# The first block's filter divided at rounding, its taps split over three engines, and other orders for tiles 0 to 30

## The chip, the cores and the metric

One core of one Trainium2 chip runs the whole program. The metric is the device time of one execution in microseconds (us); lower is better. The program is written out instruction by instruction for each engine: TensorE (PE; its weight loads are PEld), VectorE (DVE), ScalarE (ACT), GpSimd (POOL) and SyncE (SP, which issues most DMAs). Each engine runs its own list in order, and semaphores tie the lists together.

## What is computed

A short causal filter over the sequence, whose seven taps per head are a softmax, then two feed-forward layers with gates of their own:

```python
w = np.exp(weight - max); w = w / (np.sum(w, axis=-1, keepdims=True) + 1e-09)   # 8 heads x 7 taps
x = filter of x with w, causal, over S = 4096 for B = 2 sequences, D = 192      # 8192 tokens x 192
h = x @ w_in                                   # layer 1: 192 -> 2048
g = h * np.clip(h + 3.0, 0.0, 6.0) / 6.0
x = g @ w_out                                  # 2048 -> 192
h = x @ w_in2                                  # layer 2: 192 -> 2048
P = a[0] + a[1]*h + a[2]*h**2 + a[3]*h**3
Q = 1.0 + abs(b[0])*abs(h) + abs(b[1])*h**2
out = (P / (Q + 1e-6)) @ w_out2                # 2048 -> 192
```

## The kernel before, in words

The 8192 tokens are 16 blocks of 512, and features stand on the partitions. The 192 features are split into 128 (part a) and 64 (part b). A layer has 16 tiles of 128 hidden features per block, so each layer has 256 tiles. Every float32 operand of a product is kept as a rounded high part and a remainder (`_hi`, `_lo`): one ACT copy rounds, and a subtraction on POOL or DVE gives the remainder. A tile is five matmuls of 512 columns into the hidden features (`in_product`: a high times high, a low weight times high, a high weight times low, and two for part b, whose high and low halves are stacked) and five out of them (`out_product`). 2 layers x 256 tiles x 10 = 5120 matmuls. Between the two stand the gate of layer 1 (ACT `relu1`, DVE `gate1`, ACT `g1hi`, then `g1lo` on DVE before tile 21 and on POOL after it) or the quotient of layer 2 (nine ACT, DVE and POOL operations). Four PSUM banks `h_0` to `h_3` hold hidden tiles.

Layer 2 of a block runs 20 tiles behind layer 1. Tile counters `p` (layer 1) and `s` (layer 2) advance in `course`, and for each step `run` walks a list of stages from a table: START, BEGIN, RAMP (from tile 20 on, when layer 2 joins), MIDDLE, and others at the end. An entry as `("out1", 4)` places a stage that many tiles late; the order of the entries is the order of the instructions on that engine. So the tables alone set what stands behind what.

The filter: for block 0, part a is seven taps on DVE, added one after the other into a PSUM bank that is not yet in use (`conv_a_tap`, which is `sums_a(0)`). Part b is seven half-width products on ACT (`product_b`), added on POOL (`add_lower_taps`) and DVE (`add_upper_taps`, `add_halves`). The taps are a softmax: DVE finds the maximum (L893), ACT takes the exponentials with their sum (L870), and DVE adds 1e-9, inverts and scales (`normalize`) before the first tap. Beside the taps DVE refines a square root of |b1| in small steps (`refine`), which layer 2 needs in a register. `cs_a_hi`, `cs_a_lo`, `cs_b_hi`, `cs_b_lo` split the filtered block into the parts that TensorE reads. `w_in_hi`, `w_in_lo`, `w_out_hi`, `w_out_lo` do so for the weights, chunk by chunk (two tiles each). TensorE runs eight spare products (L860) while it waits for the first block. Then tiles 0 to 3 run their three part-a matmuls first, and after them their part-b ones.

Of the kernel before, what the change touches and what calls it, by code (L numbers as in the profile page):

```python
# [11 lines left out]
P = 128  # L12
BLK = 512
# [3 lines left out]
Q_ONE = 1.0 + 1e-6  # L17

TAPS_READY = 6

SPLIT_B = 4
# [39 lines left out]
    "tensor": [("in2", 0), ("in1", 0), ("out2", 4), ("out1", 2)],  # L61
    "scalar": [("conv_a_first", AHEAD, -2), ("w_out_hi", -2), ("rsq2", 1), ("w_in_hi", -2), ("relu1", 0),
             ("rec2", 1), ("sq2", 0), ("abs2", 0), ("lin2", 0), ("g2hi", 2), ("g1hi", 0), ("cs_a_hi", AHEAD, 9)],
    "vector": [("num2", 1), ("conv_a", AHEAD, (2, 4, 3, 5, 7, 8)), ("g1lo", 2), ("num1", 1), ("g_neg", 2),
             ("gate1", 0), ("newton", 1), ("conv_b_tail", AHEAD, (9, 11, 13), 0), ("g_first", 1)],
    "gpsimd": [("x2a_lo", SUM1, -1), ("den_sum", 0), ("w_in_lo", -4), ("w_out_lo", 7), ("g1lo", 0),
# [38 lines left out]
START_END, RAMP_END, END_AT = 11, 30, 258  # L105
WARM = 8
# [10 lines left out]
def build_program(nc, x_a, x_b, taps, coefs, w_pack, out):  # L117
# [56 lines left out]
    with ExitStack() as ctx:  # L174
# [811 lines left out]
```

## Time and profile before

| what | value |
| --- | --- |
| median of 3 runs | 1207.81 us (1207.76 to 1207.96) |
| the profiled execution | 1206.88 us, of which its span 1205.1 us |
| granted TensorE clock over the span | 0.999 |
| TensorE matmul busy | 1177.9 us (98%), 5138 matmuls |
| DVE, ACT, POOL busy | 1161.2, 1169.7, 1075.7 us (96%, 97%, 89%) |
| chain that ended last | TensorE 91%, ACT 5% |

A matmul row shows about 0.39 us from start to modelled end, but back-to-back matmuls start 0.227 us apart, since they are pipelined; a wait shows as a larger distance between starts. The tables below give such starts. A busy share is an average; the stretches of the first group of rows show where TensorE had gaps.

### The profile page before, as it was taken

What the parts mean: (1) busy time and instruction counts of PE and PEld (TensorE: products, weight loads), DVE (VectorE), ACT (ScalarE), POOL (GpSimd) and SP (SyncE); (2) the same over time, 40 slices, a digit from 0 to 9 for tenths busy, and PEclk for the clock granted to TensorE, in tenths of its full rate; (3) what the DMA queues carried; (4) which work ended last, traced back from release to release, by engine and by line L of the source; (5) the groups of instructions that cost most, each with busy time, mean ns of one, the idle gap of its engine ahead of it and who ended that gap; (6) DMA issues with size and microseconds to landing.
All of it is one profiled execution on the core that took longest, in us unless ns stands there. A gap on an engine that the chain in (4) does not pass through costs nothing.

```text
span 1205.1 us, 18313 instructions
## 1 busy us (share of the span) xinstructions
PE 1177.9 (98%) x5138; PEld 963.0 (80%) x5138; DVE 1161.2 (96%) x1787; ACT 1169.7 (97%) x2233; POOL 1075.7 (89%) x832
## 2 busy tenths in 40 slices
PE   6999999999999999999999999999999999999987
PEld 5778888888888888888888888888888888888764
DVE  7899999999999999999999999999999999999898
ACT  7899999999999999999999999999999999999998
POOL 5879989999999999999899998999989999898876
PEclk9999999999999999999999999999999999999999
DMA  4400000000000000010000000000000000000000
GB/s 149 149 1 10 1 23 1 23 10 23 1 1 28 5 23 1 1 32 1 23 1 22 11 1 23 1 23 10 1 23 1 23 1 13 2 1 14 1 14 14
DMA packets 10021, 21.17 MB, mean 18 GB/s; under 512 B 1600, under 2 KB 1856, under 8 KB 9920
## 3 DMA queue, kind: packets, MB, share of 16 engines
q1 hardware_dynamic: 9632, 20.00, 5.6%
q8 instruction: 40, 0.66, 0.2%
q14 instruction: 61, 0.50, 0.1%
q10 hardware_dynamic: 288, 0.01, 0.0%
HBM read 13.72 MB, written 6.29 MB: 17 GB/s over the span
## 4 chain that ended last, share of the span: by engine, by line
PE 91%; ACT 5%; issue 2%; DVE 1%; DMA 0%; POOL 0%; ACTq 0%; DVEq 0%; POOLq 0%
PE h L321 46%; PE y0a_acc L333 5%; PE y0b_acc L339 5%; PE y0a_acc L335 5%; PE y0a_acc L334 5%; PE y0b_acc L338 5%; PE y1a_acc L333 4%; PE y1b_acc L339 4%; PE y1b_acc L338 4%; PE y1a_acc L335 4%; PE y1a_acc L334 4%; ACT g_hi L532 1%; ACT num L440 1%; ACT den L446 0%; ACT sqr L452 0%
## 5 line engine op out<-in xcount | busy, mean ns | idle before, releaser
L469 POOL TENSOR_TENSOR den<-den,sqr 128x512 f32<-128x512 f32 x246 | 360.6, 1466 | 92.8 <-ACT den L446 88.5
L526 POOL TENSOR_TENSOR g_lo<-g,g_hi 128x512 fp32r<-128x512 f32 x255 | 334.0, 1310 | 2.8 <-ACT g_hi L532 2.8
L433 POOL TENSOR_TENSOR g_lo<-r,g_hi 128x512 fp32r<-128x512 f32 x235 | 306.0, 1302 | 4.2 <-ACT g_hi L532 2.4
L463 DVE SCALAR_TENSOR_TENSOR num<-num,coef,h 128x512 f32<-128x512 f32 x246 | 183.8, 747 | 8.3
L496 DVE SCALAR_TENSOR_TENSOR h<-num,coef,h 128x512 f32<-128x512 f32 x238 | 178.1, 748 | 0.2
L458 DVE TENSOR_TENSOR num<-num,h 128x512 f32<-128x512 f32 x246 | 167.8, 682 | 9.6 <-ACT num L440 4.4
L440 ACT ACTIVATE num<-h,coef 128x512 f32<-128x512 f32 x246 | 176.2, 716 | 0.2
L473 ACT ACTIVATE rsq<-den 128x512 f32<-128x512 f32 x246 | 158.6, 645 | 11.5 <-POOL den L469 8.5
L532 ACT ACTIVATE g_hi<-g 128x512 fp32r<-128x512 f32 x255 | 168.0, 659 | 1.8 <-DVE g L503 0.4
L419 DVE SCALAR_TENSOR_TENSOR r<-r,h 128x512 f32<-128x512 f32 x235 | 160.7, 684 | 6.1 <-ACT r L412 5.0
L489 DVE SCALAR_TENSOR_TENSOR den<-den,h 128x512 f32<-128x512 f32 x238 | 161.7, 680 | 0.6 <-ACT h L485 0.3
L503 DVE SCALAR_TENSOR_TENSOR g<-den,h 128x512 f32<-128x512 f32 x238 | 161.7, 679 | 0.2
L532 ACT ACTIVATE g_hi<-r 128x512 fp32r<-128x512 f32 x235 | 156.4, 665 | 0.0
L412 ACT ACTIVATE r<-h 128x512 f32<-128x512 f32 x256 | 154.4, 603 | 1.4 <-PE h L321 1.4
L446 ACT ACTIVATE den<-h 128x512 f32<-128x512 f32 x246 | 151.4, 615 | 2.0 <-DVE g L503 2.0
L452 ACT ACTIVATE sqr<-h 128x512 f32<-128x512 f32 x246 | 149.9, 609 | 0.6
L485 ACT ACTIVATE h<-rsq 128x512 f32<-128x512 f32 x240 | 147.4, 614 | 0.9 <-DVE conv_b L463 0.2
L333 PE MATMUL y1a_acc<-g_hi,wout 128*128 128x512 f32 x254 | 100.2, 395 | 8.7 <-POOL g_lo L526 6.2
L321 PE MATMUL h<-x1a_hi,win_hi 128*128 128x512 f32 x256 | 100.4, 392 | 2.7 <-DVE g L503 2.3
L333 PE MATMUL y0a_acc<-g_hi,wout 128*128 128x512 f32 x256 | 100.1, 391 | 2.4 <-DVE g_lo L433 1.4
L321 PE MATMUL h<-x0a_hi,win_hi 128*128 128x512 f32 x256 | 100.7, 393 | 0.9 <-ACT x0a_hi L532 0.4
L321 PE MATMUL h<-x1a_lo,win_hi 128*128 128x512 f32 x256 | 100.0, 391 | 0.7 <-POOL x1a_lo L540 0.7
(151 smaller groups left out, 2982.4 us busy)
## 6 DMA issues: line engine op xcount, KB each, us to landing
stage_w<-w_pack SPq DMA_DIRECT2D x16, 448.0 KB, 3.4
raw_a<-x_a SPq DMA_DIRECT2D x16, 259.0 KB, 3.3
out<-y_a SPq DMA_DIRECT2D x16, 256.0 KB, 2.0
out<-y_b SPq DMA_DIRECT2D x16, 128.0 KB, 2.3
raw_b<-x_b SPq DMA_DIRECT2D x14, 129.5 KB, 2.7
raw_b<-x_b SPq DMA_DIRECT2D x4, 65.5 KB, 4.1
tap_ab<-taps ACTq DMA_DIRECT2D x1, 7.0 KB, 3.0
coef<-coefs ACTq DMA_DIRECT2D x1, 3.0 KB, 4.0
```

The lines of the kernel that those rows point to most:

```text
L321: mm = eng.matmul(psum, w, x[:, :], start=(i == 0), stop=(i == len(passes) - 1))
L333: eng.matmul(ya_acc[l][:, :], a_hi, g_hi[:, :], start=first, stop=False)
L433: eng.tensor_tensor(g1_lo[t % 2][:, :], gated(t)[:, :], f32(g1_hi[t % 2][:, :]), ALU.subtract).then_inc(S["g1lo"], 1)
L440: eng.activation(num_of(t), h2_of(t), ACT.Identity, bias=a2, scale=reg_a3) \
L458: eng.tensor_tensor(n, n, h2_of(t), ALU.mult).then_inc(S["num2"], 1)
L463: eng.scalar_tensor_tensor(out=n, in0=n, scalar=a1, in1=h2_of(t), op0=ALU.add, op1=ALU.mult).then_inc(S["num1"], 1)
L469: eng.tensor_tensor(den_of(t), den_of(t), sqr_of(t), ALU.add).then_inc(S["den_sum"], 1)
L489: eng.scalar_tensor_tensor(out=den_of(t), in0=den_of(t), scalar=Q_ONE, in1=quotient(t), op0=ALU.add, op1=ALU.mult).then_inc(S["newton"], 1)
L496: eng.scalar_tensor_tensor(out=raw_quotient(t), in0=num_of(t), scalar=a0, in1=quotient(t), op0=ALU.add, op1=ALU.mult).then_inc(S["g_first" ...
L503: eng.scalar_tensor_tensor(out=g2[t % 2][:, :], in0=den_of(t), scalar=2.0, in1=raw_quotient(t), op0=ALU.subtract, op1=ALU.mult) \
L526: eng.tensor_tensor(g2_lo[t % 2][:, :], g2[t % 2][:, :], f32(g2_hi[t % 2][:, :]), ALU.subtract).then_inc(S["g2lo"], 1)
L532: return eng.activation(dst, src, ACT.Copy)
```

## The change

**The first block's filter is divided later.** DVE's taps and ACT's products of block 0 use the exponentials as they are (`exp_tap`). The reciprocal of their sum is multiplied in when the filtered block is rounded (`cs_a_hi`, `cs_b_hi` as a scaled copy) and when its remainder is taken. The scaled taps go to a buffer of their own, `tap`, after that, for the other blocks.

**Two of part a's seven taps move to ACT.** `product_a` makes the products of taps 5 and 6, POOL adds them to each other (`add_products_a`), and DVE adds the pair to its five taps (`last_of_a`). Part b's seven products are shared out as three for POOL and four for DVE, where they were four and three.

**The square root leaves DVE.** It is taken by ACT in seven small steps, with the function `Abs_reciprocal_sqrt` and one correction, from tile 4 on; the three register loads come after it at tile 8.

**Spare products.** 24 instead of 8, on a tile of ones that POOL makes at the very start, so they wait no longer for weights.

**Orders.** Tiles 0 and 1 run their two high part-a passes, then their low ones; tiles 2 and 3 their low pass just before part b. SP issues the first weight chunk after part b of the input. START, BEGIN and RAMP list their stages in other orders; from tile 30 on nothing is reordered.

```diff
-TAPS_READY = 6
-SPLIT_B = 4
+SPLIT_A, SPLIT_B = 5, 3
+SUMS_READY, TAPS_READY = 5, 7
...
 RAMP = {
-    "tensor": [("in2", 0), ("in1", 0), ("out2", 4), ("out1", 2)],
+    "tensor": [("in1", 0), ("in2", 0), ("out1", 2), ("out2", 4)],
...
-START_END, RAMP_END, END_AT = 11, 30, 258
-WARM = 8
+START_END, RAMP_END, END_AT = 12, 30, 258
+WARM = 24
...
                 if t == 0:
-                    for tile in range(H_BANKS):
+                    for parts in (range(2), range(2, 3)):
+                        for tile in range(WCHUNK):
+                            first_block_weights(eng, 0, tile, "w_in_done")
+                            in_product(eng, 0, tile, h1_of(tile), split, parts)
+                    for tile in range(WCHUNK, H_BANKS):
                         first_block_weights(eng, 0, tile, "w_in_done")
-                        in_product(eng, 0, tile, h1_of(tile), split, range(3))
-                in_product(eng, 0, t, h1_of(t), split, range(3, 5)).then_inc(S["h1_done"], 1)
+                        in_product(eng, 0, tile, h1_of(tile), split, range(2))
+                rest = range(3 if t < WCHUNK else 2, 5)
+                in_product(eng, 0, t, h1_of(t), split, rest).then_inc(S["h1_done"], 1)
...
+        def product_a(eng, j):
+            if j == SPLIT_A:
+                eng.wait_ge(d_raw[0], 16)
+                eng.wait_ge(S["setup_s"], 1)
+            scaled(eng, sqr[j - SPLIT_A][:, :], raw_a[0][:, j:j + BLK], exp_tap[0][:, j:j + 1]) \
+                .then_inc(S["product_a"], 1)
+        def add_products_a(eng):
+            eng.wait_ge(S["product_a"], 2)
+            eng.tensor_tensor(sqr[0][:, :], sqr[0][:, :], sqr[1][:, :], ALU.add).then_inc(S["product_a"], 1)
+        def last_of_a(eng):
+            eng.wait_ge(S["product_a"], 3)
+            eng.wait_ge(S["conv_a_tap"], SPLIT_A)
+            eng.tensor_tensor(sums_a(0), sqr[0][:, :], sums_a(0), ALU.add).then_inc(S["conv_a_tap"], K - SPLIT_A)
...
+            if k == 0:
+                eng.wait_ge(S["setup_v"], SUMS_READY)
+                ins = scaled(eng, xa_hi[0][0][:, :], sums_a(0), tap_sum[:, 0:1])
...
+        def root_begin(eng):
+            eng.wait_ge(d_const, 16)
+            eng.activation(beta[:, :], coef[:, 4:6], ACT.Abs).then_inc(S["root"], 1)
+            eng.wait_ge(S["root"], 1)
+            eng.activation(r, b1_abs, ACT.Abs_reciprocal_sqrt, bias=B_TINY).then_inc(S["root"], 1)
...
         def registers(eng):
-            eng.wait_ge(S["root_done"], 1)
+            eng.wait_ge(S["root"], 7)
...
         @block.sync
         def _(eng):
             load_a(eng, 0)
-            load_w(eng, 0)
             for right in range(2):
                 load_b_half(eng, 0, right)
-            for c in range(1, W_STAGES):
+            for c in range(W_STAGES):
                 load_w(eng, c)
...
         @block.tensor
         def _(eng):
-            eng.wait_ge(S["wi_hi"], 1)
+            eng.wait_ge(S["ones"], 2)
+            ones = xa_hi[1][0]
             for _ in range(WARM):
-                eng.matmul(h1_of(H_BANKS - 1), win_hi[0][:, 0:P], win_hi[0][:, 0:BLK], start=True, stop=True)
+                eng.matmul(h1_of(H_BANKS - 1), ones[:, 0:P], ones[:, :], start=True, stop=True)
...
         @block.vector
         def _(eng):
...
+            eng.wait_ge(S["setup_s"], 1)
+            sums = invert(0) + invert(1)
+            for j in range(SPLIT_A):
                 conv_a_tap(eng, 0, j)
+                if j < len(sums):
+                    eng.wait_ge(*((S["setup_v"], n_own[0]) if j % 2 else (S["setup_s"], 1 + j // 2)))
+                    own(sums[j]())
...
+            last_of_a(eng)
+            for j in range(SPLIT_B + 1, K):
                 add_upper_taps(eng, j)
             add_halves(eng)
+            cs_a_lo(eng, 0)
             cs_b_lo(eng, 0)
+            for part in range(2):
+                normalize(part)
...
         @block.gpsimd
         def _(eng):
-            w_in_lo(eng, 0)
+            eng.memset(rsq[0][:, :], 1.0).then_inc(S["ones"], 1)
+            eng.wait_ge(S["ones"], 1)
+            eng.tensor_tensor(xa_hi[1][0][:, :], rsq[0][:, :], rsq[0][:, :], ALU.mult).then_inc(S["ones"], 1)
+            add_products_a(eng)
             for j in range(1, SPLIT_B):
                 add_lower_taps(eng, j)
+            w_in_lo(eng, 0)
             w_in_lo(eng, 1)
```

Where instructions stand now, at the three places of which the prediction speaks. On POOL, the start of the program before (`win_lo` are weight remainders, `num` part b's products):

```order
L540 ISA
L540 TENSOR_TENSOR win_lo<-stage_w,win_hi 128x512
L657 TENSOR_TENSOR num<-num 128x256 x3
L540 TENSOR_TENSOR win_lo<-stage_w,win_hi 128x512 x2
L540 TENSOR_TENSOR wout<-stage_w,wout 128x2x128
```

and now (`rsq` and `x1a_hi` are the buffers that hold the ones, `sqr` the two products of part a):

```order
L999 MEMSET rsq 128x512
L1001 ISA
L1001 TENSOR_TENSOR x1a_hi<-rsq 128x512
L671 TENSOR_TENSOR sqr<-sqr 128x512
L688 TENSOR_TENSOR num<-num 128x256 x2
L550 TENSOR_TENSOR win_lo<-stage_w,win_hi 128x512 x3
```

The first weight remainder moved behind the ones and three additions, and one of part b's additions left POOL. On ACT, behind the exponentials, before (`num`, `den`, `y0b_acc` take part b's products; `y1b_acc` the root):

```order
L873 ACTIVATE beta<-coef 128x2
L875 ACT_TABLE_LOAD
L875 ACTIVATE y1b_acc<-beta 128x1
L532 ACTIVATE win_hi<-stage_w 128x512
L674 ACTIVATE tap_ab<-tap_ab,tap_sum 128x7
L674 ACTIVATE num<-raw_b,tap_ab 128x256 x4
L674 ACTIVATE den<-raw_b,tap_ab 128x256
L674 ACTIVATE y0b_acc<-raw_b,tap_ab 128x256
L674 ACTIVATE den<-raw_b,tap_ab 128x256
L532 ACTIVATE x0a_hi<-y0a_acc 128x512
L532 ACTIVATE win_hi<-stage_w 128x512 x2
L532 ACTIVATE wout<-stage_w 128x2x192
```

and now:

```order
L705 ACTIVATE sqr<-raw_a,tap_ab 128x512 x2
L705 ACTIVATE num<-raw_b,tap_ab 128x256 x4
L542 ACTIVATE win_hi<-stage_w 128x512
L705 ACTIVATE y0b_acc<-raw_b,tap_ab 128x256
L705 ACTIVATE den<-raw_b,tap_ab 128x256 x2
L705 ACTIVATE x0a_hi<-y0a_acc,tap_sum 128x512
L542 ACTIVATE win_hi<-stage_w 128x512
L705 ACTIVATE x0b_hl<-y0b_acc,tap_sum 64x256 x2
L542 ACTIVATE win_hi<-stage_w 128x512
```

Three small operations and a table load left this place, two full-width products came in, and the weights' first rounding stands behind four of part b's products. On PE, at tile 20, where layer 2 begins, before (x0 is the input of layer 1, x1 that of layer 2; the first row ends the output product of tile 16):

```order
L338 MATMUL y0b_acc<-g1_hi0,wout0 128x512
L339 MATMUL y0b_acc<-g1_lo0,wout0 128x512
L321 MATMUL h_0<-x1a_hi0,win_hi1 128x512
L321 MATMUL h_0<-x1a_hi0,win_lo1 128x512
L321 MATMUL h_0<-x1a_lo0,win_hi1 128x512
L321 MATMUL h_0<-x1b_hl0,win_hi1 128x512
L321 MATMUL h_0<-x1b_hl0,win_lo1 128x512
L321 MATMUL h_3<-x0a_hi1,win_hi0 128x512
L321 MATMUL h_3<-x0a_hi1,win_lo0 128x512
L321 MATMUL h_3<-x0a_lo1,win_hi0 128x512
L321 MATMUL h_3<-x0b_hl1,win_hi0 128x512
L321 MATMUL h_3<-x0b_hl1,win_lo0 128x512
```

and now:

```order
L343 MATMUL y0b_acc<-g1_hi0,wout0 128x512
L344 MATMUL y0b_acc<-g1_lo0,wout0 128x512
L326 MATMUL h_3<-x0a_hi1,win_hi0 128x512
L326 MATMUL h_3<-x0a_hi1,win_lo0 128x512
L326 MATMUL h_3<-x0a_lo1,win_hi0 128x512
L326 MATMUL h_3<-x0b_hl1,win_hi0 128x512
L326 MATMUL h_3<-x0b_hl1,win_lo0 128x512
L326 MATMUL h_0<-x1a_hi0,win_hi1 128x512
L326 MATMUL h_0<-x1a_hi0,win_lo1 128x512
L326 MATMUL h_0<-x1a_lo0,win_hi1 128x512
L326 MATMUL h_0<-x1b_hl0,win_hi1 128x512
L326 MATMUL h_0<-x1b_hl0,win_lo1 128x512
```

The five matmuls of layer 1's tile 20 changed places with those of layer 2's tile 0, and so it goes on for every tile up to 29.

## Rows read from the trace of the kernel before

**Rows 1.** Busy time by stretch: span, PE, PEld, DVE, ACT, POOL (count), PE clock, DMA.

```profile
19.20:56.00 36.80, 36.49 (x158) 29.35 (x158) 32.27 (x50) 30.46 (x61) 29.36 (x34) 1.00 0.49 153
56.00:78.00 22.00, 18.99 (x80) 14.38 (x80) 20.55 (x33) 20.80 (x39) 13.94 (x12) 1.00 0.07 27
78.00:1140.00 1062.00, 1061.87 (x4677) 876.91 (x4676) 1035.93 (x1582) 1045.29 (x1993) 975.62 (x735) 1.00 0.04 11
```

**Rows 2.** Order of time, 0 to 11 us: start, length, engine, line, operation, [idle <-releaser].

```profile
0.24 0.10 POOL L979 MEMSET const-float32-0.0<- 128x1 f32 x1 [0.24 <-issue]
...
4.43 0.15 DVE L900 TENSOR_SCALAR tap_sum<-tap_sum 128x1 f32<-128x1 f32 x1 [0.46 <-ACT tap_ab L870]
...
5.08 0.75 DVE L675 TENSOR_SCALAR y0a_acc<-raw_a,tap_ab 128x512 f32<-128x512 f32 x1
...
7.53 3.48 PE L860 MATMUL h<-win_hi 128*128 128x512 f32 x8 [7.53 <-ACT win_hi L532]
...
7.55 1.28 POOL L540 TENSOR_TENSOR win_lo<-stage_w,win_hi 128x512 fp32r<-128x512 f32 x1 [7.11 <-ACT win_hi L532]
...
7.76 1.71 ACT L674 ACTIVATE num<-raw_b,tap_ab 128x256 f32<-128x256 f32 x4
...
8.78 2.48 POOL L657 TENSOR_TENSOR num<-num 128x256 f32<-128x256 f32 x3
```

**Rows 3.** Order of time, 11 to 16 us.

```profile
11.42 0.47 PE L321 MATMUL h<-x0a_hi,win_hi 128*128 128x512 f32 x1 [0.41 <-ACT x0a_hi L532]
...
11.91 0.42 DVE L664 TENSOR_TENSOR y0b_acc<-y0b_acc,den 128x256 f32<-128x256 f32 x1
...
13.73 0.86 DVE L538 SCALAR_TENSOR_TENSOR x0b_hl<-y0b_acc,x0b_hl 64x256 fp32r<-64x256 f32 x2 [0.84 <-ACT x0b_hl L532]
...
14.72 0.42 PE L321 MATMUL h<-x0b_hl,win_hi 128*128 128x512 f32 x1
...
15.41 1.09 ACT L412 ACTIVATE r<-h 128x512 f32<-128x512 f32 x2 [0.80 <-PE h L321]
```

**Rows 4.** Order of time, 16 to 22 us: the first output product.

```profile
16.38 0.72 ACT L674 ACTIVATE conv_a<-raw_a,tap_ab 128x512 f32<-128x512 f32 x1
...
18.41 0.68 DVE L433 TENSOR_TENSOR g_lo<-y1a_acc,g_hi 128x512 fp32r<-128x512 f32 x1
...
19.23 0.47 PE L333 MATMUL y0a_acc<-g_hi,wout 128*128 128x512 f32 x1 [0.95 <-POOL wout L540]
...
22.02 0.50 PE L333 MATMUL y0a_acc<-g_hi,wout 128*128 128x512 f32 x1 [0.27 <-DVE g_lo L433]
```

**Rows 5.** Waits of ScalarE, 20 to 55 us: total, times, longest.

```profile
ACT g_hi L532 <- PE y0b_acc L339: 4.6, 8, 1.2
```

**Rows 6.** Order of time, 54 to 60 us: the second layer begins.

```profile
54.35 0.60 ACT L546 ACTIVATE y_a<-y0a_acc 128x512 f32<-128x512 f32 x1 [0.54 <-PE y0b_acc L339]
...
56.93 0.50 PE L338 MATMUL y0b_acc<-g_hi,wout 128*128 128x512 f32 x1 [0.80 <-DVE x1b_hl L572]
...
58.42 0.70 DVE L419 SCALAR_TENSOR_TENSOR y1b_acc<-r,h 128x512 f32<-128x512 f32 x1
...
59.18 0.50 PE L321 MATMUL h<-x0a_hi,win_hi 128*128 128x512 f32 x1 [0.35 <-DVE y1b_acc L419]
```

**Rows 7.** Order of time, 63 to 76 us: both layers together.

```profile
63.78 1.28 ACT L473 ACT_TABLE_LOAD   x1
...
65.08 0.63 ACT L473 ACTIVATE rsq<-den 128x512 f32<-128x512 f32 x1
...
66.23 0.69 DVE L419 SCALAR_TENSOR_TENSOR r<-r,h 128x512 f32<-128x512 f32 x1 [0.80 <-ACT r L412]
...
69.64 0.50 PE L333 MATMUL y0a_acc<-g_hi,wout 128*128 128x512 f32 x1 [1.08 <-DVE g_lo L433]
...
75.14 0.68 DVE L419 SCALAR_TENSOR_TENSOR r<-r,h 128x512 f32<-128x512 f32 x1
...
75.36 0.47 PE L321 MATMUL h<-x1a_hi,win_hi 128*128 128x512 f32 x1 [0.78 <-DVE g L503]
```

More of the change, by code:

```diff
@@ L224, in build_program @@
         tap_ab = sb("tap_ab", 2 * K)
-        tap = [tap_ab[:, i * K:(i + 1) * K] for i in range(2)]
+        exp_tap = [tap_ab[:, i * K:(i + 1) * K] for i in range(2)]
+        tap_rows = sb("tap", 2 * K)
+        tap = [tap_rows[:, i * K:(i + 1) * K] for i in range(2)]
         tap_max, tap_sum = sb("tap_max", 2), sb("tap_sum", 2)
@@ L649, in product_b @@
                 eng.wait_ge(d_raw_b0, 32)
[L650 to L651 removed]
+                eng.wait_ge(S["setup_s"], 2)
+            scaled(eng, products[j], raw_b[:, j:j + HALF], exp_tap[1][:, j:j + 1]).then_inc(S["product_b"], 1)
         def add_lower_taps(eng, j):
@@ L817, in run @@
                 for stage, lag, *at in plan[name]:
+                    if stage in once:
+                        if p >= lag and stage not in placed:
+                            placed.add(stage)
+                            once[stage](eng)
+                        continue
                     if stage in tiles1 or stage in tiles2:
@@ L869, in _ @@
             for part in range(2):
-                eng.activation(tap[part], tap[part], ACT.Exp, bias=tap_max[:, part:part + 1],
+                eng.activation(exp_tap[part], exp_tap[part], ACT.Exp, bias=tap_max[:, part:part + 1],
                                accum_out=tap_sum[:, part:part + 1]).then_inc(S["setup_s"], 1)
-            eng.wait_ge(d_const, 16)
-            eng.activation(beta[:, :], coef[:, 4:6], ACT.Abs).then_inc(S["setup_s"], 1)
-            eng.wait_ge(S["setup_s"], 3)
-            eng.activation(root_steps[0], b1_abs, ACT.Sqrt).then_inc(S["setup_s"], 1)
+            for j in range(SPLIT_A, K):
+                product_a(eng, j)
+            for j in range(4):
+                product_b(eng, j)
             w_in_hi(eng, 0)
-            eng.wait_ge(S["setup_v"], TAPS_READY)
-            scaled(eng, tap[1], tap[1], tap_sum[:, 1:2]).then_inc(S["setup_s"], 1)
-            for j in range(K):
+            for j in range(4, K):
                 product_b(eng, j)
@@ L928, in _, with invert, normalize @@
-            cs_a_lo(eng, 0)
-            for j in range(SPLIT_B + 2, K):
+            def invert(part):
+                guarded = yb_acc[1][:, 2 + part:3 + part]
+                return [lambda: eng.tensor_scalar(guarded, total[part], 1e-9, None, ALU.add),
+                        lambda: eng.reciprocal(total[part], guarded)]
+            def normalize(part):
+                eng.wait_ge(S["setup_v"], SUMS_READY)
+                own(eng.tensor_scalar(tap[part], exp_tap[part], total[part], None, ALU.mult))
```

123 lines of the change are left out of this document (62 added, 61 removed).

## Prediction

> **What bounds the kernel now.** I read the busy times by stretch first [rows 1]. From 78 to 1140 us TensorE is busy 1061.87 of 1062.00 us: it sets the time, and no order of the other engines gains anything there. The last 65 us are the end of the program, whose orders stay. What is left lies before. Until 11.42 us no real product has started [rows 3], and up to the one at 19.23 there are waits between them [rows 3, 4]. From 19.2 to 56 TensorE is full again (36.49 of 36.80 us), and from 56 to 78 it is idle 22.00 - 18.99 = 3.0 us. As TensorE is full for 1062 us behind these stretches, each microsecond by which it gets through them earlier comes off the end. So I follow three marks: the first output product (19.23 us), the second (22.02 us) [rows 4], and the join with layer 2, until 78 us.
>
> The next view was the order of time in these stretches, for what each mark waits for. Back-to-back matmuls start 0.227 us apart (1061.87 us over 4677 matmuls), so ten of them, a tile's two products, take 2.27 us.
>
> **The start, step by step.** Times are from the start of the span.
>
> DVE: the sum of the exponentials is there at 4.43 us, and the first tap started only at 5.08 [rows 2], behind three small operations. These go, so the first tap starts at 4.43: 0.65 earlier. Five taps of 0.75 plus some 0.04 each end at 8.4 instead of seven at 10.6.
>
> ACT, with no table load and no root in its way, starts the two products of part a at 4.7, behind the second exponential, some 0.3 us after the first sum. The nearest row for one is the scaled copy of 128x512 in 0.72 us [rows 4]; bounds are 0.55 (half of the 1.09 us of two plain copies [rows 3]) and 0.75 (a DVE tap). I take 0.72, with starts 0.62 apart: ready at 6.0. Then come four half-width products, the first weight rounding and three more; four took 1.71 us [rows 2], so 0.40 apart. That gives 5.9 to 7.5, 7.5 to 8.05 and 8.05 to 9.3.
>
> POOL: the pair of part a is added from 6.1. The nearest row is the subtraction of 128x512 in 1.28 us [rows 2], so 7.4, well before DVE's 8.4. Then two additions of 2.48 / 3 = 0.83 us each [rows 2] until 9.1, and the first weight remainder (1.28) until 10.4. Before, that remainder was POOL's first work and ended at 8.8; it is now what comes last before the first real product.
>
> DVE adds the pair (0.7, between the 0.42 of a half-width addition and 0.75) until 9.1, and ACT rounds from 9.3 to 9.9. So the first real product starts at 10.45, when the weight remainder is there, 0.97 earlier. Four high passes run to 11.4. DVE meanwhile needs four half-width additions, 0.42 plus a hand-over, about 0.52 each [rows 3], until 11.15; part a's remainder, which is queued behind them, ends at 11.9. TensorE waits 0.6 for it: this is the wait that the new order adds. Two low passes then, and four high ones of tiles 2 and 3 until 13.35.
>
> Part b: ACT rounds from 11.2 to 12.0 (0.84 before), DVE takes the remainder in 0.86 until 12.9 [rows 3]. TensorE comes at 13.35, against 14.72 before. ACT's first gate step followed 0.69 behind that start (15.41 [rows 3]) and so comes at 14.0: 1.4 earlier.
>
> From there to the first output product DVE is the queue: gate (0.7) until 15.35; a tap of block 1, which waits until ACT's scaled copy ends at 15.7; second gate until 17.15; remainder of tile 0 (0.68) until 17.95. In the old order it ended at 19.09 [rows 4]. The first output product starts at 18.1 instead of 19.23. The second waits in both for the next remainder; now four DVE operations stand between (gate 0.7, one scaled copy 0.4 and two half-width taps, together 1.0 to 1.4), which gives 21.0 instead of 22.02 [rows 4]. **Gain at the start: 1.0 us.** Ends: 0.5, if ACT's third weight rounding has to wait for the chunk that is loaded again; 1.7, if the second output product doesn't wait at all.
>
> The spare products end before they are needed, if POOL can start at once: a fill of 128x512 (between 0.10, the small fill at POOL's start [rows 2], and 1.28) and a product (1.28) from 0.75 us on: the ones are there between 2.1 and 3.3. The eight before took 3.48 us [rows 2], 0.43 apart; the next ones ran 0.23 apart. The granted level rose from 1.2 to 2.4 GHz while they ran. The other 16 then take 3.6, so the end is between 9.2 and 10.4, before 10.45. A pause of about a microsecond does not lower the clock here: after one of 0.95 us [rows 4] the products ran 0.23 apart again.
>
> **Tiles 4 to 15.** ACT gets one table load (1.28 [rows 7], some 0.2 more since what stands before it must end first), six tiny steps that each wait for the last (0.3 each) and register loads of 0.4: about 3.9 us that were not here. In this stretch ACT waited 4.6 us for TensorE to free a buffer, eight times, never over 1.2 at once [rows 5]. The load is below what is idle, so I count nothing; the single step that is longer than a wait (1.46 against 1.2) is covered since the rounded tile is ready some 0.9 us before its product. If the cover fails it costs up to 1.5.
>
> In the Trainium skill, "ScalarE: Activation LUTs", section "What ACT_TABLE_LOAD costs", a switch is a load of 1.28 us and a drain of 1.38. The load agrees with the trace; the drain does not show, since the next activation starts at 65.08, 0.02 us behind the load's end [rows 7]. By the page's 2.66 ACT's extra work would be 5.1 us and the rival below on ACT likelier.
>
> **The join with layer 2.** Call T the moment at which ACT can move block 0's result (54.35 before [rows 6]). TensorE's next stall ended at T + 2.58 (56.93). In the new order the result of part a comes behind a rounding (T + 1.6, a stall of 0.65 at a product that had none), part b's behind a gate and a remainder (T + 2.65): nothing gained, 0.1 lost. But the gate of tile 19 stands right after it (T + 3.3; it was 58.42 + 0.70, or T + 4.8), and layer 1's tile 20 goes before layer 2's tile 0, so TensorE waits 0.2 in place of the stall that ended at 59.18 (0.35 idle, 0.53 by starts). Both tiles end at T + 5.6 instead of T + 6.0: 0.35 gained.
>
> Then the table load at 63.78 is gone, and tile 21's product stands before layer 2's tile 1, so ACT's gate step no longer waits. The chain of DVE reaches the gate of tile 21 at T + 10.35, not 66.23 = T + 11.88 [rows 7]: 1.5 earlier. From this gate to the remainder that TensorE waited for it is 69.6 - 66.2 = 3.4 us of DVE work in the same order, so the product at 69.64 (T + 15.3) starts at T + 13.95: 1.35 gained, with 0.35 of the 1.08 us of idle time left. After that DVE's loop takes (75.14 - 66.23) / 2 = 4.46 us per pair of tiles, just under TensorE's 20 x 0.227 = 4.53. Layer 1's product, now first, needs the gate, which is later than what layer 2's needs: I find stalls of 0.5 and 0.95 in place of the 0.93 that ended at 75.36. **Kept: 1.15 us**, between 0.4 and 2.6 (the 3.0 us of idle less at least 0.4 of new waits). DVE is then 0.4 us further ahead than TensorE; of the small gaps behind it I count 0.3 as closed (0 to 0.6).
>
> **The sum.** 1.0 + 1.15 + 0.3 = 2.45 us. The profiled execution took 1206.88 us (span 1205.1 and 1.8 around it), so it becomes 1204.4; the median of the runs is 0.93 above it, which makes 1205.3 of 1207.81.
>
> **Rivals.**
> - *The join gives nothing.* DVE and ACT are busy 20.6 and 20.8 of 22.0 us there [rows 1], near their limit; if the new order only moves the waits, the start's 1.0 stays: 1206.8. For it: the product that needs the gate is now first. Against it: 1.28 us of ACT work really leaves. 10%.
> - *ACT overruns at tiles 6 to 10.* 3.9 us against 4.6 is close, and the root's steps wait for each other. It would give back 1.5: 1206.8. 8%.
> - *The join gives nearly all.* If the second-layer stalls close (2.6) and the start gives 1.4: 1203.8. 20%.
> - *GpSimd is late with the ones (slower).* Before, POOL shows nothing from 0.4 to 7.55 us [rows 2], so a start-up cost of its first real operation could hide there. Were its first result still only there at 8.8, the 24 spare products would hold TensorE until 15.9, where the high passes can start as late as 11.05 without loss: 4.85 lost, 2.45 gained, so 1210.2. It decides from ones later than 3.9 us, and turns the change slower from 6.4 on. Against it: the fill at 0.24 us shows POOL at work [rows 2]. 7%. "GPSIMD Engine Reference" of the Trainium skill, section "Instruction dispatch", says that the first call of freshly loaded kernel code pays about 6 us; by it the ones come at 8.4 and the time at 1209.8. No row here can show it.
>
> **How the numbers follow.** The forecast has 55%, its own range 1204.2 to 1206.2. 0.2%, about what a measurement of this kernel can tell from no change, is 2.4 us, a time of 1205.4, so the forecast lies on this border; with more ways to gain at the join than I counted I give it 0.36 beyond and 0.19 within. Faster: 0.36 + 0.20 = 0.56. Same: 0.19 + 0.10 + 0.08 = 0.37. Slower: 0.07. The range goes to 1203.3 below (start 1.7, join 2.6, rest 0.2) and 1207.2 above (start 0.6 alone), and leaves out the slower case and little of the ends.
>
> **What would show it.** First real product at 10.3 to 10.7 us, with the weight remainder as its releaser, and then a wait of 0.6 for part a's remainder; first output product near 18.1, second near 21.0; no gap from 23 to 52 us; the table load around 22 us and none at 62; at 56 to 78 about 2 us idle instead of 3.0, the wait at the first product of layer 1's tiles 23 and 24. A first real product after 11.1 with spare products before it, or new waits of TensorE for ACT at 25 to 40 us, would make the forecast wrong.

## The result and the profile after

The kernel after takes 1205.28 us (median of 13 runs, 1205.19 to 1205.75); the kernel before took 1207.96 beside it (13 runs, 1207.56 to 1208.70). The ratio is 0.9978, 95% interval 0.9970 to 0.9987: 0.22% faster, just past the 0.2% that the forecast took as the border; the interval goes from 0.13% to 0.30%. Beside the last experiments it was 1204.90 against 1207.35, which is 2.45 us, the forecast's sum. The forecast was 1205.3.

The profiled execution took 1205.52 us with a span of 1203.7, only 1.36 less than the one before (1206.88), while the medians differ by 2.68. That one execution of before lies 1.08 below its median; this one lies 0.24 above. So spans of single executions can't settle a difference of 2 us here; the marks in the next part are compared inside the first 160 us.

The busy times by stretch, same columns as [rows 1]:

```profile
19.20:56.00 36.80, 35.66 (x155) 28.53 (x153) 32.97 (x51) 33.36 (x71) 31.48 (x35) 1.00 0.51 165
56.00:78.00 22.00, 20.47 (x85) 15.69 (x86) 20.67 (x33) 20.53 (x40) 16.25 (x14) 1.00 0.03 9
78.00:1140.00 1062.00, 1061.55 (x4675) 876.06 (x4674) 1035.76 (x1581) 1045.38 (x1991) 973.19 (x734) 1.00 0.04 11
```

From 56 to 78 us TensorE is idle 1.5 us instead of 3.0. But one of the join's waits (0.60) and part of a second now fall before 56, which is most of why the first row went from 36.49 to 35.66. A border that waits can cross misleads: the join has to be followed by marks of its own.

The start, in order of time, against [rows 2] and [rows 3]:

```profile
0.73 0.52 POOL L999 MEMSET rsq<- 128x512 f32 x1 [0.29 <-POOLq L1045]
...
1.33 1.04 POOL L1001 TENSOR_TENSOR x1a_hi<-rsq 128x512 fp32r<-128x512 f32 x1
...
2.43 7.39 PE L935 MATMUL h<-x1a_hi 128*128 128x512 f32 x24 [2.43 <-POOL x1a_hi L1001]
...
4.53 0.75 DVE L706 TENSOR_SCALAR y0a_acc<-raw_a,tap_ab 128x512 f32<-128x512 f32 x1 [0.46 <-ACT tap_ab L945]
...
4.68 1.32 ACT L705 ACTIVATE sqr<-raw_a,tap_ab 128x512 f32<-128x512 f32 x2
...
8.92 1.28 POOL L550 TENSOR_TENSOR win_lo<-stage_w,win_hi 128x512 fp32r<-128x512 f32 x1
...
10.26 0.50 PE L326 MATMUL h<-x0a_hi,win_hi 128*128 128x512 f32 x1 [0.45 <-POOL win_lo L550]
...
12.04 0.70 PE L326 MATMUL h<-x0a_lo,win_hi 128*128 128x512 f32 x2 [0.59 <-DVE x0a_lo L548]
```

and up to the second output product, against [rows 4]:

```profile
14.22 3.83 POOL L550 TENSOR_TENSOR wout<-stage_w,wout 128x256 fp32r<-128x256 f32 x6
...
17.35 0.69 DVE L443 TENSOR_TENSOR g_lo<-y1a_acc,g_hi 128x512 fp32r<-128x512 f32 x1
...
18.18 0.47 PE L338 MATMUL y0a_acc<-g_hi,wout 128*128 128x512 f32 x1 [0.94 <-POOL wout L550]
...
21.16 0.50 PE L338 MATMUL y0a_acc<-g_hi,wout 128*128 128x512 f32 x1 [0.42 <-DVE g_lo L443]
```

The ones are there at 2.42 us, the 24 spare products end at 9.82, the first real product starts at 10.26 on the weight remainder, and the new wait of 0.59 for part a's remainder follows. The first output product comes 1.05 earlier than before, the second 0.86. The profile puts the wait before the first one down to POOL's remainders of the output weights, as it did before [rows 4]. They end at 18.05 us, and DVE's remainder of tile 0, which the forecast followed, at 18.04.

ScalarE while TensorE is full, the first rows of the root:

```profile
24.14 1.28 ACT L827 ACT_TABLE_LOAD   x1
25.43 0.20 ACT L827 ACTIVATE root<-beta 128x1 f32<-128x1 f32 x1
```

and its waits from 20 to 55 us (total, times, longest), against [rows 5]:

```profile
ACT r L422 <- PE h L326: 0.9, 3, 0.5
...
ACT g_hi L542 <- PE y0b_acc L344: 0.6, 1, 0.6
```

Of the 4.6 us for which it waited for TensorE's output products 0.6 is left, and TensorE did not feel it: from 22 to 54 us no two of its matmuls start more than 0.26 us apart.

The join, against [rows 6] and [rows 7]:

```profile
53.26 0.60 ACT L542 ACTIVATE x1b_hl<-y0b_acc 64x512 fp32r<-64x512 f32 x1
53.33 0.70 DVE L429 SCALAR_TENSOR_TENSOR y1a_acc<-r,h 128x512 f32<-128x512 f32 x1
...
54.23 0.58 ACT L556 ACTIVATE y_a<-y0a_acc 128x512 f32<-128x512 f32 x1
...
54.96 0.47 PE L338 MATMUL y0a_acc<-g_hi,wout 128*128 128x512 f32 x1 [0.60 <-ACT y_a L556]
...
56.24 0.50 PE L343 MATMUL y0b_acc<-g_hi,wout 128*128 128x512 f32 x1 [0.35 <-DVE x1b_hl L582]
...
64.07 0.69 DVE L429 SCALAR_TENSOR_TENSOR r<-r,h 128x512 f32<-128x512 f32 x1
...
67.66 0.50 PE L338 MATMUL y0a_acc<-g_hi,wout 128*128 128x512 f32 x1 [0.18 <-DVE g_lo L443]
...
69.51 0.51 PE L326 MATMUL h<-x0a_hi,win_hi 128*128 128x512 f32 x1 [0.41 <-DVE r L429]
...
73.88 0.50 PE L326 MATMUL h<-x0a_hi,win_hi 128*128 128x512 f32 x1 [0.69 <-DVE r L429]
```

The table load at 63.78 is gone and tile 20's output product comes 1.98 earlier (69.64 to 67.66), but two waits for gates follow it (0.57 and 0.85 by starts).

### The profile page after: what moved, and what is told of

It reads as the page before. It is cut to its first block, busy times and chain, and to the rows that moved or that the text cites. A ratio compares the mean times of both kernels' runs of the same rounds, so it can differ in the third digit from the quotient of the medians.

```text
span 1203.7 us, 18353 instructions
## 1 busy us (share of the span) xinstructions
PE 1181.9 (98%) x5154; PEld 966.3 (80%) x5154; DVE 1162.2 (97%) x1782; ACT 1171.1 (97%) x2238; POOL 1078.9 (90%) x834
## 4 chain that ended last, share of the span: by engine, by line
PE 85%; ACT 5%; DVE 5%; issue 3%; POOL 0%; DMA 0%; ACTq 0%; DVEq 0%; POOLq 0%
PE h L326 43%; PE y0b_acc L343 4%; PE y0a_acc L338 4%; PE y0b_acc L344 4%; PE y0a_acc L340 4%; PE y0a_acc L339 4%; PE y1a_acc L338 4%; PE y1b_acc L344 4%; PE y1b_acc L343 4%; PE y1a_acc L339 4%; PE y1a_acc L340 4%; ACT g_hi L542 1%; DVE g L513 1%; DVE num L468 1%; ACT num L450 1%
```

## The marks used below

The same product can be looked up in every trace: the start of layer 1's output product of tile 14 (in the full stretch), 20 and 24 (in the join) and 40 (behind all tables that differ). The numbers are the gain against the kernel before in us, from one profiled execution each, worked out from the third matmul of the product less 0.45. In kernels with the new order of TensorE tile 24's product also stands five matmuls (1.13 us) earlier in the program; that is taken off. Before, the four stood at 50.76, 69.76, 87.93 and 160.57 us. The last column is the difference of the medians.

| kernel | tile 14 | tile 20 | tile 24 | tile 40 | medians |
| --- | --- | --- | --- | --- | --- |
| after | 1.10 | 1.97 | 1.44 | 2.42 | 2.68 |
| after, again | 1.12 | 2.02 | 1.50 | 2.45 | 2.45 |
| start alone | 1.21 | 1.63 | 1.61 | 1.59 | 1.27 |
| orders alone | -2.61 | -2.68 | -3.22 | -2.28 | -1.56 |
| layer 2 first | 1.26 | 0.83 | 0.82 | 1.28 | 0.99 |
| table load alone | -0.26 | 0.13 | 0.14 | 0.08 | 0.22 |
| old BEGIN, new RAMP | 1.15 | 1.05 | 0.51 | 0.81 | 0.74 |
| sum before the tap | 0.61 | 1.51 | 0.98 | 1.96 | 1.81 |
| 8 spare products | -1.14 | -0.24 | -0.80 | 0.17 | 0.09 |
| 16 spare products | 1.25 | 2.13 | 1.59 | 2.56 | 2.49 |
| 40 spare products | -1.56 | -0.68 | -1.21 | -0.24 | -1.10 |
| part b together | 1.19 | 2.14 | 1.59 | 2.53 | 2.53 |

Except for "orders alone" and "40 spare products" (of which more below) the gain at tile 40 is within 0.35 us of the medians'. That fits the forecast's argument that the time is won or lost before 160 us, but the traces alone do not prove it. In the same traces, all but "orders alone", the gain at the last matmul of the program is smaller than at tile 40, by up to 1.06 us: for the kernel after it is 1.36 (1201.18 against 1199.82), for its second execution 1.87. Small gaps make up most of that difference. Between 165 and 1030 us the kernel after has eight of them, 0.84 us in all; this execution of before has one, of 0.07 us. "Table load alone", nearly the same program, has five, so this trace of before, which also lies 1.08 below its median, is probably a lucky one; no second trace of that kernel was kept.

## The experiments

**Start alone.** The kernel after with the tables of before; only the root's steps are added to START.

```diff
-    "tensor": [("in1", -2), ("out1", 2)],
+    "tensor": [("in1", 0), ("out1", 4)],
...
-    "tensor": [("in1", 0), ("in2", 0), ("out1", 2), ("out2", 4)],
+    "tensor": [("in2", 0), ("in1", 0), ("out2", 4), ("out1", 2)],
...
-START_END, RAMP_END, END_AT = 12, 30, 258
+START_END, RAMP_END, END_AT = 11, 30, 258
...
```

> The changed start (taps divided later, two ACT products, spare products, the root on ACT from tile 4) with the old order tables for tiles 0 to 30. Theory A, that at the join with layer 2 it is ScalarE's table load whose leaving brings the gain: first output product near 18.2 us, gate of tile 21 about 2 us earlier than before, 1.8 to 2.5 us faster than before in all. Rival B, that the new orders bring the join's gain: the start's 0.9 us alone, 0.7 to 1.1 us faster.

Measured: 1206.23 us (1206.12 to 1206.43) against 1207.50, ratio 0.9988 (0.9979 to 0.9997). It lies between the two ranges. The marks say why: 1.21 at tile 14 is the start, 0.40 more comes at the join, and nothing after it. Its first two output products, with the old order, start at 17.83 and 20.35, earlier than in the kernel after (18.18 and 21.16): the new START order does not help there.

**Orders alone.** The kernel before with the BEGIN and RAMP of after.

```diff
...
-    "vector": [("conv_b_head", PAIR_AHEAD, (16, 16, 17), 0), ("x2b_lo", SUM1, 0), ("gate1", 0),
+    "vector": [("cs_b_lo", AHEAD, -12, 1), ("conv_b_head", PAIR_AHEAD, (14, 17, 17), 0), ("gate1", 0),
...
-    "tensor": [("in2", 0), ("in1", 0), ("out2", 4), ("out1", 2)],
+    "tensor": [("in1", 0), ("in2", 0), ("out1", 2), ("out2", 4)],
...
```

> The kernel before with the changed order tables for tiles 11 to 30 alone (start as before, table load still at 62 to 64 us). Theory A: the join stays as slow, within 0.4 us of before. Rival B: 1.2 to 1.8 us faster.

Measured: 1209.06 us (1208.85 to 1209.44), ratio 1.0012 (1.0003 to 1.0021): 1.56 slower, which neither theory had. The trace has two reasons. One is a wait in a stretch that was full. On VectorE the remainder of the next block's part b, which the new BEGIN takes one tile earlier, holds the queue for 2.00 us (0.86 for the pair in [rows 3]), and TensorE waits for the hidden tile's remainder behind it:

```profile
40.67 1.29 POOL L539 TENSOR_TENSOR win_lo<-stage_w,win_hi 128x512 fp32r<-128x512 f32 x1
40.68 2.00 DVE L537 SCALAR_TENSOR_TENSOR x0b_hl<-conv_b,x0b_hl 64x256 fp32r<-64x256 f32 x2 [0.29 <-ACT x0b_hl L531]
...
43.32 0.68 DVE L432 TENSOR_TENSOR g_lo<-y1a_acc,g_hi 128x512 fp32r<-128x512 f32 x1
...
44.15 0.47 PE L332 MATMUL y0a_acc<-g_hi,wout 128*128 128x512 f32 x1 [1.76 <-DVE g_lo L432]
```

The wait is 1.93 by starts. Of the two halves of the pair the first took 1.56 us instead of 0.42; POOL's subtraction ran beside it from its first moment. In the kernel after the same pair takes 0.85 from 39.91 us on, with POOL idle beside it, and the wait is not there. That the neighbour makes the operation slow fits these rows; it was not tested, nor whether START's new order or the changed start keeps the two apart. The second reason is not the edit's: 0.73 us at the first output product, in this execution (see the section on the hardware). Less that, the loss at tile 40 is 1.55, as in the medians.

**Layer 2 first.** The kernel after, with TensorE's line of RAMP as before.

```diff
-    "tensor": [("in1", 0), ("in2", 0), ("out1", 2), ("out2", 4)],
+    "tensor": [("in2", 0), ("in1", 0), ("out2", 4), ("out1", 2)],
```

> The changed kernel with one line of the RAMP table put back: on TensorE layer 2's products stand ahead of layer 1's for tiles 20 to 29. By my prediction the new order brings 0.3 us or so at tile 20 and turns the wait for a quotient into one for a gate: 0 to 0.5 us slower than the changed kernel (2.2 to 2.7 us faster than before). Rival: the order is what closes the stall at tile 20's output product, by the earlier gate of tile 21: more than 0.8 us slower than the changed kernel.

Measured: 1206.51 us (1205.97 to 1206.71), ratio 0.9991 (0.9982 to 1.0000): 1.0 below before, where the kernel after is 2.45 to 2.68 below. The rival was right: with the rest of the new orders in place, this one line is worth 1.1 us at tile 40 and 1.5 to 1.7 in the medians. TensorE's waits in the trace:

```profile
58.06 0.50 PE L326 MATMUL h<-x1a_lo,win_hi 128*128 128x512 f32 x1 [0.79 <-POOL x1a_lo L550]
...
68.81 0.50 PE L338 MATMUL y0a_acc<-g_hi,wout 128*128 128x512 f32 x1 [0.66 <-DVE g_lo L443]
...
74.52 0.47 PE L326 MATMUL h<-x1a_hi,win_hi 128*128 128x512 f32 x1 [0.77 <-DVE g L513]
```

Layer 2's first product meets a remainder that POOL now makes later (0.95 by starts), and the 0.93 at layer 2's product comes back. At tile 24 the new order of TensorE is worth 0.62, from there to tile 40 another 0.52.

**Table load alone.** The kernel before with one tiny use of the root function at tile 4, so that the load at 63.78 is gone.

```diff
...
+            eng.activation(root[:, 1:2], beta[:, 0:1], ACT.Abs_reciprocal_sqrt, bias=Q_ONE)   # at tile 4
...
```

> The kernel before plus one tiny Abs_reciprocal_sqrt activation on ScalarE at tile 4 (its result is not used), so that the table is loaded near 24 us and no longer at 63.8 us. Theory A: 0.8 to 1.6 us faster than before, the output product of tile 20 about 1 us earlier, and the gaps between 100 and 125 us closed. Rival B: within 0.3 us of before.

Measured: 1207.28 us (1207.01 to 1207.84), ratio 0.9998 (0.9989 to 1.0007). The rival was right on the time. At the join it gains 0.40 (tile 14 to 24), of a load of 1.28, and behind it nothing. The rows show what is late next; before, ScalarE's step started at 65.61 and the gate at 66.23 [rows 7]:

```profile
65.46 0.60 ACT L412 ACTIVATE r<-h 128x512 f32<-128x512 f32 x1 [0.92 <-PE h L321]
...
66.09 0.69 DVE L419 SCALAR_TENSOR_TENSOR r<-r,h 128x512 f32<-128x512 f32 x1 [0.40 <-ACT r L412]
```

ScalarE stands idle 0.92 us for TensorE's hidden tile and the gate comes only 0.4 earlier (this execution runs 0.27 later by its start). With the old orders two thirds of the load's time are not to be had.

**Eight, forty and sixteen spare products.** Each is the kernel after with one number changed.

```diff
-WARM = 24
+WARM = 8        # 40 and 16 in the two others
```

> The changed kernel with 8 spare products instead of 24. They end near 5.9 us, and TensorE then has nothing until 10.26. Theory: the clock has fallen to its lower level by then, the first products start 0.43 us apart again until about 13.5 us, the first gate step comes 0.5 to 1.0 us later and the kernel is 0.5 to 1.0 us slower than the changed one (1.7 to 2.2 faster than before). Rival: the clock stays up over the pause and the time is that of the changed kernel (2.7 faster than before).

Measured with 8: 1207.56 us (1206.94 to 1208.67) against 1207.65, ratio 0.9999 (0.9990 to 1.0008). Nearly the whole gain is gone. In its trace the spare products end at 6.21 and the real ones start as early as with 24:

```profile
10.10 0.80 PE L326 MATMUL h<-x0a_hi,win_hi 128*128 128x512 f32 x1 [3.88 <-POOL win_lo L550]
10.69 0.63 PE L326 MATMUL h<-x0a_hi,win_lo 128*128 128x512 f32 x1
11.12 0.63 PE L326 MATMUL h<-x0a_hi,win_hi 128*128 128x512 f32 x1
...
15.36 0.39 PE L326 MATMUL h<-x0b_hl,win_hi 128*128 128x512 f32 x1
```

They come 0.43 us apart until 15.08, then 0.23. ScalarE's first gate step moves from 14.14 to 15.55 and the second output product from 21.16 to 23.39. Neither the theory nor the rival had the size: my 0.5 to 1.0 was too small, since I counted the products and not what hangs behind them. The theory also had the wrong reason. The trace's own record of the granted level begins at 15.16 us, with the full one; with 24 spare products it begins at 5.98. So the level did not fall in the pause: as far as these records go, with eight spare products, which started 0.42 or more apart, it had not risen before it.

> The changed kernel with 40 spare products. They end near 13.4 us, and the first real products can start as late as 11.05 us without loss. Theory of my slower rival's price: one microsecond for each beyond 11.05, so 2.2 to 2.5 us slower than the changed kernel, 0.2 to 0.5 faster than before. Rival: later waits (1.1 us at 18.2, 0.6 at 21.2) absorb part of it: under 1.5 us slower than the changed kernel.

Measured with 40: 1208.75 us (1207.62 to 1209.48), ratio 1.0008 (0.9999 to 1.0017). Both expectations missed: it is 3.5 to 3.8 above the kernel after in the medians, where the theory had 2.2 to 2.5. The first real product starts at 13.09 instead of 10.26, 2.83 later, of which 2.66 are left at tile 40. The profiled execution is the fastest of the eleven, with the median 1.1 above it. In it the level rose at 5.55 us; in the second execution of the kernel after it rose at 7.60, with 16 spare products at 7.79. Two microseconds more at 0.43 apart would let the 40 products end some 1.0 us later (my estimate from these distances). That would be enough, but the other ten executions left no trace.

> The kernel after with 16 spare products instead of 24. They end near 8.0 us (eight at 0.43 and eight at 0.23 us from 2.4 us on), so a pause of 2.3 us stands before the first real product, where 24 leave 0.4 and 8 left 3.9. Theory (a pause of this length lowers the rate like the long one): the first real products come 0.43 us apart as with 8, and the time is 1.2 to 2.1 us above the kernel after. Rival (only the long pause does it, the shorter one leaves the rate at 0.23 us): the first real product starts at the same time, and the time is within 0.2 us of the kernel after.

Measured with 16: 1204.86 us (1204.70 to 1207.21) against 1207.35, ratio 0.9981 (0.9972 to 0.9990), the same as the kernel after on that chip; one of the eleven runs took 1207.21, which stays open. My theory was wrong, the rival right on the time:

```profile
2.43 6.41 PE L935 MATMUL h<-x1a_hi 128*128 128x512 f32 x16 [2.43 <-POOL x1a_hi L1001]
10.10 0.50 PE L326 MATMUL h<-x0a_hi,win_hi 128*128 128x512 f32 x1 [1.26 <-POOL win_lo L550]
10.44 0.39 PE L326 MATMUL h<-x0a_hi,win_lo 128*128 128x512 f32 x1
10.67 0.40 PE L326 MATMUL h<-x0a_hi,win_hi 128*128 128x512 f32 x1
```

Behind a pause of 1.26 us the products run 0.23 apart. The level had risen at 7.79 us, within the spare products. The last eight spare products of the kernel after are not needed here.

**The sum before the tap.** The kernel after with three small operations on DVE ahead of the first tap, as the old order had them, each waiting for the last.

```diff
             eng.wait_ge(S["setup_s"], 1)
+            own(eng.tensor_scalar(yb_acc[1][:, 4:5], total[0], 1e-9, None, ALU.add))
...
+            own(eng.reciprocal(yb_acc[1][:, 5:6], yb_acc[1][:, 4:5]))
...
+            own(eng.tensor_scalar(yb_acc[1][:, 8:8 + K], exp_tap[0], yb_acc[1][:, 5:6], None, ALU.mult))
...
```

> The changed kernel with the three small VectorE operations (add, reciprocal, scale) put back ahead of the first tap; their results are not used. Theory: VectorE's chain is what part a's remainder and part b stand behind, so all of the 0.65 us comes back: 0.5 to 0.65 us slower than the changed kernel. Rival: the first block waits for weights and POOL, and it costs under 0.2 us.

Measured: 1205.84 us (1205.46 to 1205.97) against 1207.65, ratio 0.9986 (0.9977 to 0.9995). The first tap starts at 5.04 instead of 4.53, and 0.5 us is missing at tile 14 and still at tile 40: what DVE loses there, everything loses. The theory was right; in the medians it is 0.6 to 0.9.

```profile
5.04 0.76 DVE L706 TENSOR_SCALAR y0a_acc<-raw_a,tap_ab 128x512 f32<-128x512 f32 x1
...
10.65 0.47 PE L326 MATMUL h<-x0a_hi,win_hi 128*128 128x512 f32 x1 [0.95 <-ACT x0a_hi L705]
```

**Old BEGIN, new RAMP.** "Start alone" with the RAMP of after.

```diff
-    "tensor": [("in2", 0), ("in1", 0), ("out2", 4), ("out1", 2)],
+    "tensor": [("in1", 0), ("in2", 0), ("out1", 2), ("out2", 4)],
...
```

> The changed start with the old START and BEGIN tables, and of the new tables only RAMP (tiles 20 to 29, layer 1's products first). Theory: RAMP alone brings the join's gain, since the old START waits less at the second output product (0.14 against 0.59 us): 1206.23 - 1.3 = as fast as the changed kernel or up to 0.3 us faster, 2.5 to 3.0 us faster than before. Rival: BEGIN and RAMP belong together, as the orders on the old start showed (1.5 us slower than before): less than 1.8 us faster than before.

Measured: 1206.91 us (1206.82 to 1208.50), ratio 0.9998 (0.9989 to 1.0007); four of the eleven runs lie 1.2 to 1.7 us above the other seven, which I can't explain. The rival was right. The first product of tile 20 stands ahead of layer 2's and runs into a gate that in the old BEGIN stands one gate and one remainder further behind part b's remainder on DVE (1.68 by starts; 0.16 in the kernel after):

```profile
55.75 0.70 DVE L430 SCALAR_TENSOR_TENSOR y1a_acc<-r,h 128x512 f32<-128x512 f32 x1
...
58.02 0.50 PE L327 MATMUL h<-x0a_hi,win_hi 128*128 128x512 f32 x1 [1.51 <-DVE y1b_acc L430]
```

**Part b together.** The kernel after, with the two steps for which TensorE waits at 54.96 and 56.24 moved ahead of a rounding and of a remainder.

```diff
-    "scalar": [("y1a_out", SUM1, 1), ...  ("x2b_hi", SUM1, 0), ...
+    "scalar": [...  ("x2b_hi", SUM1, 0), ("y1a_out", SUM1, 0), ...
-             ("x2b_res", SUM1, 0), ("g1lo", 1), ("x2b_lo", SUM1, 0), ...
+             ("x2b_res", SUM1, 0), ("x2b_lo", SUM1, 0), ("g1lo", 1), ...
```

> The kernel after, with one change at the join: ScalarE moves block 0's result of part a directly behind the rounding of part b, and VectorE takes part b's remainder before the remainder of the hidden tile, so that both of TensorE's waits near 55 us (0.76 and 0.51 by starts) should shrink. Theory (the join gained less than forecast because of the order at its first stalls): y_a comes 0.5 us earlier, part b's remainder 0.6 earlier, the stalls shrink by 0.3 to 0.9 and 0.1 to 0.5 us of it stays at the end: faster than the kernel after by that. Rival (VectorE's queue sets the join: the gate of tile 21 and the output product of tile 20 come when VectorE's work is done, and it has the same work): the first stalls shrink, those at 67.7, 69.5 and 73.9 grow by as much, and the time is within 0.1 us of the kernel after.

Measured: 1204.82 us (1204.70 to 1205.39) against 1207.35, ratio 0.9979 (0.9970 to 0.9988); the kernel after beside it 1204.90. The rival was right:

```profile
54.38 0.47 PE L338 MATMUL y0a_acc<-g_hi,wout 128*128 128x512 f32 x1
...
55.44 0.51 PE L343 MATMUL y0b_acc<-g_hi,wout 128*128 128x512 f32 x1
...
56.21 0.70 DVE L429 SCALAR_TENSOR_TENSOR y1b_acc<-r,h 128x512 f32<-128x512 f32 x1
...
56.96 0.50 PE L326 MATMUL h<-x0a_hi,win_hi 128*128 128x512 f32 x1 [0.78 <-DVE y1b_acc L429]
```

The two waits shrink from 0.76 and 0.51 by starts to 0.28 and 0.29, and the next product waits 0.95 instead of 0.16, for a gate that starts at 56.21 as before (56.22). Three waits of 1.43 became three of 1.52. VectorE's queue sets the time here: the same four operations, one right behind the other from 53.3 us on, stand in front of that gate in both kernels, only in another order.

**The kernel after again.**

> The kernel after, unchanged, on the same chip and beside the same runs of the kernel before as the two others, so that they can be compared with it directly. Expected 2.4 to 2.7 us below the kernel before (1205.28 against 1207.96 on its first chip); a gain under 2 us would say that the difference depends on the chip.

Measured: 1204.90 us (1204.68 to 1205.15) against 1207.35, ratio 0.9979 (0.9970 to 0.9988). The gain repeats, and its marks are within 0.06 of the first execution's. None of the variants is faster than the kernel after by more than 0.1 us.

## Why the forecast was right, step by step

**The start (1.0 forecast).** Shown: 1.05 and 0.86 at the first two output products, 1.10 at tile 14, and 1.21 with the start alone. The steps held too: first tap 4.53 (4.43), pair of part a 0.66 per product (0.72), first real product 10.26 (10.45), the added wait 0.59 (0.6), output products 18.18 and 21.16 (18.1 and 21.0). One path was missing from it: POOL's output-weight remainders end together with DVE's remainder (18.05 and 18.04), and before they were the last to end (19.22 against 19.09). So by these rows a gain on DVE alone would not have moved the first output product, and the forecast did not look at that. The experiment that gives back DVE's 0.5 us loses 0.5 at every mark and 0.6 to 0.9 in the medians.

**The ones (2.1 to 3.3 us forecast).** 2.42. The rival on a late GpSimd is ruled out: its second operation took 1.04 us at 1.33. "GPSIMD Engine Reference" of the Trainium skill, section "Instruction dispatch", has some 6 us for the first call of freshly loaded code; by that the ones would have come at 8.4, and this trace does not show it.

**The spare products' worth (not in the sum).** I showed only that 24 do no harm. With eight, as before, the change would have brought 0.09 us and not 2.45: eight products that start at 2.43 end at 6.21, before the granted level had risen, and the real ones behind them ran 0.43 us apart for 5 us. A part that I had costed at nothing carries the gain of the others. The experiments show that 16 and 24 do it and that 40 are too many.

**Tiles 4 to 15 (0 forecast).** Right: ScalarE's idle time took the load and the root. (The terms of the extra work, 1.28 + 0.2 + six times 0.3 + 0.4, add up to 3.7 us and not 3.9.)

**The join (1.15 forecast).** This term was mis-sized: from tile 14 to tile 24 the gain grew by 0.34, not 1.15. There are two parts to it. T is ScalarE's first step of block 0's result, 53.26 now.

The first part, about 0.45, is DVE's queue at the first waits. Between T and the gate that the next product needs stand four operations: a gate, the rest of part b, a hidden tile's remainder and part b's remainder. Each takes 0.69 or 0.70 with 0.03 in between. So the product that waits for part b's remainder comes at T + 2.98 and not T + 2.65, and the gate behind it ends at T + 3.66 and not T + 3.3. The gate of tile 21 follows at T + 10.81 (forecast T + 10.35) and tile 20's output product at T + 14.40 (T + 13.95). "Part b together" changed the order of the first waits: they moved and nothing was gained, so the limit is DVE's amount of work in front of that gate.

The second part, about 0.3, is arithmetic. The forecast's own terms do not give 1.15: 1.35 at tile 20's product, less what the later waits grow by (0.5 + 0.95 against 0.93), is 0.83. T + 10.35 and 3.4 also make T + 13.75, not T + 13.95. The later waits were forecast well: 0.57 and 0.85.

Where the 0.34 comes from is shown too. The table load moved away gives 0.40 there by itself, and "start alone", with the old orders, also 0.40. So up to tile 24 the new orders together gain nothing beyond the load.

**The small gaps behind it (0.3 forecast).** From tile 24 to tile 40 it is 0.98. From 88 to 160 us the kernel before has nine places where two matmuls of TensorE start more than 0.25 us apart, 1.10 us over the usual distance in all. These rows show one (0.42 instead of 0.23). The kernel after has two, 0.24 in all.

```profile
111.76 0.39 PE L339 MATMUL y1b_acc<-g_lo,wout 128*128 128x512 f32 x1
112.18 0.50 PE L321 MATMUL h<-x0a_hi,win_hi 128*128 128x512 f32 x1
```

"Start alone" and "table load alone" gain nothing there, so it comes from the new orders. It needs them together: BEGIN and RAMP on the old start gain 0.94, RAMP without BEGIN 0.30, and both without TensorE's line of RAMP 0.46. Which moves of the other engines count was not tried.

The two errors, 0.8 too much and 0.7 too little, cancel. The sum, 2.42 at tile 40 against 2.45, is right partly by luck, and that the spare products sufficed was luck as well; the start is right by its mechanism, but for POOL's path.

**The rivals.** "The join gives nothing" was nearer for tiles 20 to 24 than I had it, but the orders paid later, between tiles 24 and 40. ScalarE's overrun and the late GpSimd did not occur. "The join gives nearly all" did not either.

## What to carry to other kernels

- Follow one product through every trace, in front of, within and behind the changed stretch: it says where time is won at 0.1 us, when medians only say how much.
- An engine's order is worth something only with the orders around it: the new BEGIN and RAMP lost 1.6 us on the old start, and with the new START they brought 1.2 to 1.4 on the new one. START's share was not tried by itself.
- When the first real work of TensorE moves, ask whether the products that run ahead of it still bring it to the full rate: here eight no longer did, and it cost the whole gain.
- Add up a forecast's terms once more before the sum: here 0.3 us of the 0.8 by which one term was off was in the adding.

## What the runs showed of the hardware

**The column of the granted clock at the start.** It shows 1.00 in all rows here, also where the products come 0.43 us apart, the distance of the 1.2 GHz level. In the run with 8 spare products (span, busy time and count of PE, PEld, DVE, ACT, POOL, then the clock, DMA share and rate):

```profile
12.00:14.00 2.00, 2.00 (x6) 1.61 (x6) 1.78 (x3) 1.60 (x4) 1.13 (x1) 1.00 0.00 0
```

Six matmuls in 2 us where 0.23 apart would be nine: the distance between starts tells the level, the column does not. The trace's records of the level say why: the first one, of the full level, begins at 15.16 us in this run, and the column counts what lies before the first record as full. The records agree with the distances: they begin at 5.98 us with 24 spare products (7.60 in the second execution), 7.79 with 16 and 15.16 with 8, and the distance of 0.43 ends at 6.00, 7.71 and 15.08. With eight, TensorE ran them at the lower level, paused 3.88 us and then ran another twelve real products before the level rose. No run here has a pause this long after the level has risen; behind pauses of 1.26 (16 spare products) and 0.45 (24) it stayed.

**Eight spare products were on the edge.** In the kernel before they took 3.48 us, the level rose at 10.52, and the real ones behind them ran mostly 0.23 apart. In "orders alone", whose start is the same, they took 3.78, and the next products came 0.43 apart until the level rose at 13.64:

```profile
7.84 3.78 PE L859 MATMUL h<-win_hi 128*128 128x512 f32 x8 [7.84 <-ACT win_hi L531]
11.73 0.76 PE L320 MATMUL h<-x0a_hi,win_hi 128*128 128x512 f32 x1
12.29 0.63 PE L320 MATMUL h<-x0a_hi,win_lo 128*128 128x512 f32 x1
```

Its first output product is 0.73 us late, so that much differs from one execution to the next with no change in this part of the code. It may be part of why the kernel before varies more (1207.56 to 1208.70) than the one after (1205.19 to 1205.75); that was not tested.

**GpSimd at once.** A fill of 128x512 took 0.52 us and a product of that size 1.04, both less than the 1.28 of the subtraction that I had taken as their upper bound.
